# One list of block moves per head pair, with sources and targets that change partition halves from each move to the next

## The reference

```python
scores = scale * np.matmul(q, k.transpose(0, 1, 3, 2))            # 4 x 8 heads, 576 x 576, head size 64
thresh = np.max(scores, axis=-1, keepdims=True) - tau
scores = np.where(scores >= thresh, scores, -1000000000.0)
attn = softmax(scores)                                            # denominator + 1e-09
x = attn @ v                                                      # -> 2304 x 512 tokens
g = leaky(x @ w_in, alpha); x = g @ w_out                         # 512 -> 2048 -> 512
out = ((x @ w1) * (x @ w2)) @ w3 @ w_out                          # 512 -> 1024 -> 1024 -> 512
```

## Time and profile before

| | |
|---|---|
| median of 3 runs | 1059.97 us |
| profiled execution | 1060.03 us, its span 1058.1 us |
| TensorE busy (matmul) | 990.3 us, 94% |
| VectorE, ScalarE, GpSimd busy | 519.6, 420.0, 472.2 us |
| DMA | 156.39 MB; SyncE's queue 37.3% and ScalarE's 10.8% of 16 engines' span |

### The profile page before, as it was taken

The page is one execution under the profiler, slowest core; times in us unless marked ns, Lnnn a source line. Parts: engine busy times, 40 slices in busy tenths (PEclk is TensorE's granted clock), DMA queues, the critical chain, the costliest instruction groups (busy, mean ns, idle before and its releaser), DMA issues.

```text
span 1058.1 us, 18205 instructions
## 1 busy us (share of the span) xinstructions
PE 990.3 (94%) x6848; PEld 899.6 (85%) x6848; DVE 519.6 (49%) x1374; ACT 420.0 (40%) x1000; POOL 472.2 (45%) x580
## 2 busy tenths in 40 slices
PE   3799956999999999999999999999999999999998
PEld 2566634777877787889999999999999999999998
DVE  6888977899998998922332222222111111111111
ACT  5666655666665666434323333333111111211210
POOL 5877768766666656323444444444212111111211
PEclk9799986999999999999999999999999999999999
DMA  7389898787878686768153222263211011011000
GB/s 261 86 242 276 263 302 199 197 229 185 234 196 237 184 208 181 198 168 300 56 198 131 113 112 113 112 250 133 91 68 45 24 68 46 23 68 46 24 23 24
DMA packets 53224, 156.39 MB, mean 148 GB/s; under 512 B 8208, under 2 KB 20496, under 8 KB 49424
## 3 DMA queue, kind: packets, MB, share of 16 engines
q1 hardware_dynamic: 42144, 122.78, 37.3%
q10 hardware_dynamic: 10992, 32.45, 10.8%
HBM read 79.05 MB, written 32.51 MB: 105 GB/s over the span
## 4 chain that ended last, share of the span: by engine, by line
PE 61%; DVE 13%; DMA 7%; POOL 5%; issue 5%; ACT 4%; SPq 4%; ACTq 1%; POOLq 0%
PE psum L693 19%; PE psum L726 19%; PE psum L679 11%; PE psum L638 5%; DVE nmx L940 5%; DMA zbuf<-ybuf 4%; DVE e_ring L953 4%; PE psum L600 3%; SPq L443 3%; POOL g L1069 2%; PE psum L651 2%; PE psum L583 2%; DVE g_raw L985 1%; ACT g_raw L840 1%; DMA k_raw<-k 1%
## 5 line engine op out<-in xcount | busy, mean ns | idle before, releaser
L1069 POOL TENSOR_TENSOR g<-g_raw,g 128x288 fp32r<-128x288 f32 x192 | 158.7, 831 | 378.8 <-ACT g L922 235.1
L726 PE MATMUL psum<-xy,w_a 128*128 128x288 f32 x1536 | 206.1, 295 | 0.6 <-DVE y_buf L1053 0.6
L726 PEld LDWEIGHTS psum<-xy,w_a 128*128 128x128 f32 x1536 | 205.2, 188 | 0.8 <-DVE y_buf L1053 0.8
L583 PE MATMUL psum<-ks,qs 128*128 128x288 f32 x640 | 121.4, 320 | 37.3 <-DVE e_ring L953 25.3
L583 PEld LDWEIGHTS psum<-ks,qs 128*128 128x128 f32 x640 | 101.2, 204 | 53.9 <-DVE e_ring L953 35.5
L1098 POOL TENSOR_SCALAR e_ring<-e_ring,rden,uni 128x576 f32<-128x576 f32 x144 | 118.6, 825 | 60.3 <-DVE rden L964 56.8
L805 ACT ACTIVATE e_ring<-psum,nmx 128x576 f32<-128x576 f32 x144 | 106.7, 741 | 82.1 <-DVE nmx L940 82.0
L985 DVE SCALAR_TENSOR_TENSOR g_raw<-g_raw,beta_sb,psum 128x288 f32<-128x288 f32 x128 | 65.7, 514 | 127.2 <-ACT g_raw L840 127.0
L953 DVE SCALAR_TENSOR_TENSOR e_ring<-psum,thr,e_ring 128x576 f32<-128x576 f32 x144 | 115.4, 801 | 12.4 <-ACT e_ring L805 11.9
L600 PE MATMUL psum<-zbuf,vs 128*64 128x320 f32 (+1 forms) x640 | 107.9, 433 | 13.7 <-DMA zbuf<-ybuf 10.9
L940 DVE TENSOR_REDUCE nmx<-psum 128x1 f32<-128x576 f32 x144 | 108.5, 753 | 22.7 <-PE psum L583 22.3
(11 more groups left out here) (53 smaller groups left out, 1105.7 us busy)
## 6 DMA issues: line engine op xcount, KB each, us to landing
zbuf<-ybuf SPq DMA_DIRECT2D x96, 180.0 KB, 4.4
raw_a<-weights SPq DMA_DIRECT2D x56, 256.0 KB, 6.9
zbuf<-ybuf SPq DMA_DIRECT2D x96, 144.0 KB, 4.3
xy<-xs SPq DMA_DIRECT2D x12, 1152.0 KB, 5.2
q_raw<-q ACTq DMA_DIRECT2D x16, 576.0 KB, 6.2
xs<-x_hl SPq DMA_DIRECT2D x32, 288.0 KB, 6.1
ys<-xy SPq DMA_DIRECT2D x8, 1152.0 KB, 4.4
xy<-ys SPq DMA_DIRECT2D x8, 1152.0 KB, 5.1
```

The costliest lines, as they stand in the source:

```text
L583: last = mm(dst, qs[:, par, at:at + P], ks[:, par, part, h, cols], start=(m == 0), stop=(m == 2 * len(terms) - 1))
L726: last = mm(psum[:, 2 * ab + f % 2, 0:CH], w_a[:, wp, slot, (f % 4) * P:(f % 4 + 1) * P], xy[c][:, xp, kt, :], start=(n == 0), stop=(n == ...
L1069: sub = lambda out_, a, hi: nc.gpsimd.tensor_tensor(out_, a, hi.bitcast(F32), ALU.subtract)
```

## The change

The moves of a pair stand in two lists of (source group, target group). SyncE's queue issues the twelve moves of the first list together in step `LAG_MOVE`, after one wait for `s_t` and for both `s_pv`. ScalarE's queue issues the four of the second list in the same four steps as before. The same sixteen blocks are moved, each once, and each `y` keeps its semaphore.

```diff
+SP_MOVES = [(0, 0), (2, 2), (0, 1), (2, 3), (1, 0), (3, 2), (0, 2), (2, 0), (0, 3), (2, 1), (1, 1), (3, 3)]
+ACT_MOVES = [(1, 2), (1, 3), (3, 0), (3, 1)]
...
-            def move_blocks(n, y):
+            def move_blocks(n):
                 sp.wait_ge(s_t, TILES * (n + 1))
                 if n >= 1:
-                    sp.wait_ge(s_pv[y], n)
-                for k in range(QD):
-                    dst, src = move(n, 2 * y, (2 * y + k) % QD)
-                    sp.dma_start(dst, src).then_inc(s_z[y], 16)
-                    if k % 2 == 1:
-                        dst, src = move(n, 2 * y + 1, (2 * y + 3 + k // 2) % QD)
-                        sp.dma_start(dst, src).then_inc(s_z[y], 16)
+                    for y in range(2):
+                        sp.wait_ge(s_pv[y], n)
+                for a, c in SP_MOVES:
+                    sp.dma_start(*move(n, a, c)).then_inc(s_z[a // 2], 16)
...
-                for y in range(2):
-                    if pair_at(s, LAG_MOVE + y) is not None:
-                        move_blocks(pair_at(s, LAG_MOVE + y), y)
+                if pair_at(s, LAG_MOVE) is not None:
+                    move_blocks(pair_at(s, LAG_MOVE))
...
-            def move_blocks(n, y, half):
+            def move_blocks(n, m):
+                a, c = ACT_MOVES[m]
                 act.wait_ge(s_t, TILES * (n + 1))
                 if n >= 1:
-                    act.wait_ge(s_pv[y], n)
-                dst, src = move(n, 2 * y + 1, (2 * y + 1 + half) % QD)
-                act.dma_start(dst, src).then_inc(s_z[y], 16)
+                    act.wait_ge(s_pv[a // 2], n)
+                act.dma_start(*move(n, a, c)).then_inc(s_z[a // 2], 16)
...
-                for y in range(2):
-                    for half in range(2):
-                        if pair_at(s, LAG_MOVE + 2 * y + half) is not None:
-                            move_blocks(pair_at(s, LAG_MOVE + 2 * y + half), y, half)
+                for m in range(len(ACT_MOVES)):
+                    if pair_at(s, LAG_MOVE + m) is not None:
+                        move_blocks(pair_at(s, LAG_MOVE + m), m)
```

## The result

The changed kernel took 1112.23 us, the median of four runs (1109.69 to 1115.85), against 1059.51 us for the kernel before in the same comparison. The ratio is 1.0497 with a 95% interval of 1.0461 to 1.0532: slower by 53 us. The profiled execution of the changed kernel (1115.85 us) is the slowest of its four, 3.6 us above their median, so its rows add up to a little more than the 53 us. I had forecast 1049.0 us, in a range of 1042 to 1063 us.

The account below looks back on a forecast made before the run. TensorE was taken as the bound, VectorE at about 145 to 185 us, moves mattering only where these wait. Terms -5.8 - 3.75 - 2.2 - 0.5 + 1.0 = -11.25 us against 1060.03 gave 1049 us, range 1042 to 1063.

Parts of the forecast that it names:

- The issue of twelve moves: SyncE's queue, each pair: 7.3 us, taken as 8.5, in place of 12.7; what stands behind goes out 4.2 us earlier.
- The weight load of pair 3: Behind pair 3's moves on SyncE's queue: lands at 144.8 us, cutting VectorE's 6.83 us wait to about 1.0, gain 5.8 us.
- y = 1: Lands some 13 us after the first move; gives back 3.75 us in pair 4, 2.2 in pairs 1, 10 and 14.
- y = 0: Last move now eleventh, landing at 10.1 us, inside 10.7: no charge in middle pairs, 0.5 us gain in pair 0.
- half rate stays, and y = 0 is late: Rival: moves stay at 200 GB/s, TensorE waits 40 us at y = 0; +30 us, 1090 us; chance 0.11.
- The wait for both products: SyncE's wait for `s_pv[1]` before its first move: matters in pair 15 alone, charged 1.0 us, free in other pairs.
- The rule that I set aside: Skill's 6% gain for two transfers in opposite halves: rate some 212 GB/s, time that of the half-rate rival.

Follow-up runs that it names:

- e7: Changed kernel with y = 0 from source groups 0 and 2, y = 1 from 1 and 3, y = 0 first, halves alternating: 1047.32 us, ratio 0.9891.
- e1: Changed kernel, its single list and wait kept, but in the order of the kernel before, all y = 0 moves first: 1059.38 us, ratio 1.0009.
- m1: Only block moves, no attention or feed-forward, in separate stages on SyncE's queue: 16 moves took 16.3 us lower to lower, 14.0 us with both halves changing.
- m2: Only SyncE's twelve moves, in changed order and order before, without and with a 576 KB load: y = 0 landed at 9.5, 13.6, 6.7 and 8.7 us.
- e4: Changed kernel with ScalarE's load of the next pair's keys issued two steps later: 1079.29 us, ratio 1.0183.
- e6: Changed kernel with all products of values one step later (LAG_PV + 1): 1092.48 us, ratio 1.0316.
- e9: e7 with a list that changes the source half once in three moves: 1053.6 us, ratio 0.9921.

## Why the prediction was wrong

**The issue of twelve moves** was forecast at 7.3 to 8.5 us, with 12.7 as the bound; it took 10.56 us in pair 8. Over all pairs it fell from 11.4 to 9.4 us on average. Right in sign, too small.

**The weight load of pair 3** hardly holds ScalarE up any more (0.3 us in place of 7.93), and VectorE's long wait behind it is gone. That looks like my term of 5.8 us, but only part of it is. I had the load landed 17.2 us after the pair's first move (144.8 less 127.59). It landed at 19.2 us, where it was 23.0 before, and in this pair TensorE stood 7.34 us at y = 0, so that ScalarE came to the piece only 2.4 us after it had landed. e7 shows the load without that: it lands at 19.8 us, and ScalarE still waits for it:

```profile
145.15 0.62 ACT L782 CAST w_a<-raw_a 128x512 fp32r<-128x512 f32 x1 [4.80 <-DMA raw_a<-weights]
```

That is 3.1 us less than before, and VectorE's longest wait is 3.1 us shorter as well (3.7 in place of 6.83). So the term is about 3 us and not 5.8. e1, where the wait is back at 7.7 us, shows that merging the two lists alone gives nothing here.

**y = 1** is waited for nowhere, as forecast, though in pair 8 it lands 17.6 us after the first move, no earlier than before: the late y = 0 covers it. I had 13 us.

**y = 0 is the step that failed.** I had its last move issued at 6 us, 2.6 us to its landing and 1.5 us for the keys, 10.1 us, "just inside 10.7 us, so I charge nothing". That compared a lower bound with the deadline and put the wait of TensorE at the first products at nothing. It landed at 16.9 us in pair 8, and the idle time before the products grew by 48.0 us. Three sizes were wrong. The move went out at 7.4 us, since the queue still backs up. The rate was 239 GB/s in pair 13: I took 303 GB/s in a 0.7 us window as the rate of a list, and m1 gives 257 at best. And the keys weren't 1.5 us: m2 has 4.1 us for the same load beside the mixed order, and e4 33 us of kernel time for it. Rows 6 could have warned me: a shortest landing of 2.6 us beside a median of 4.5 and a longest of 9.4 us says that in traffic the shortest isn't the one to take for a move that stands eleventh.

**The rival** "half rate stays, and y = 0 is late" had the mechanism, the place and a threshold of 240 GB/s, just above the measured rate, and got 0.11. It charged the load of keys with 1.5 us too, had 40 us of waits at y = 0 where 61.7 came, and left out the clock, 12.9 us, though the products after a wait in pair 4 took 1.19 us for four of the narrow form before as well, against 0.76 elsewhere. A margin of 0.6 us in even pairs against a delay that hangs on what else is in the queues deserved far more than that.

**The wait for both products** costs nothing that can be told: e1 has it too. In pair 15, where I charged 1.0 us, the changed kernel waits 4.17 us, but e1 doesn't wait there for y = 0 at all.

**The rule that I set aside.** The Trainium skill (SBUF — State Buffer, "Can I just issue two DMAs to hit both halves?") gives +6% for two transfers in opposite halves. In m1 only a change of both sides shortened a stage, by 14% for 180 KB moves and 6% for the 324 KB ones (14.7 to 13.8 us); in the kernel the rate rose by a tenth. That is much nearer to the rule than to my 50%.

## What to carry to other kernels

When a batch of transfers serves two consumers, the time that counts is the landing of the last transfer that the first consumer waits for. Here interleaving the two raised the rate by a tenth and gave the first consumer nearly the finish of the whole batch; it was better to regroup the work so that the interleaved transfers all belong to the first consumer. And before a list is reordered, look at what another queue issues in its midst: here one load of 576 KB, two steps later, was worth 33 us in one order and 4 in the other.

## What the runs showed of the hardware

- SBUF-to-SBUF moves of 32 partitions run at 202 to 209 GB/s, moves over all 128 at 423, with the DMA engines fully busy in both (m1). Of m1's lists only those in which both source and target change halves take less time, 14.0 in place of 16.3 us for 16 moves of 180 KB, at 255 to 257 GB/s in their steady part.
- With a load of 576 KB from another queue beside them, the waited-for moves landed 2.0 to 4.1 us later (m2), more than the 1.5 us that its bytes take at 400 GB/s.
- A wait of TensorE can cost more than its length. After eleven of the thirteen waits of the changed kernel (2.12 to 9.00 us) the first eight products took 1.83 to 2.37 us; after the other two (1.02 and 2.01 us), and after one of 2.94 us in e6, they took 1.26 us. The mean granted clock over the profiled span was 0.959 in place of 0.982, and the same 6848 matmuls took 12.9 us longer.
- Why two neighbours in one list that change both sides take less time in m1, and why a list without such a turn gained too in e9, stays open.
